# Four narrow bias tables moved from ScalarE to VectorE, and the wide tables placed earlier in ScalarE's order

## What is computed

```python
scores = scale * np.matmul(q, k.transpose(0, 1, 3, 2))       # B=2, H=8, S=768, D=64
keep = is_global | is_local                                  # first 8 keys, or 0 <= rel < 96
dist = np.where(is_global & ~is_local, float(n_local), np.abs(rel).astype(np.float32))
slopes = 2.0 ** (-8.0 * (np.arange(H) + 1) / H)
scores = scores - slopes[:, None, None] * dist               # then masked, softmax, times v
# x = attention output as (B, S, 512)
# block 1: u = x + (U V mixing over tokens); y = u + relu(u @ w_ch1) @ w_ch2
# block 2: h = relu(y @ w_in); half of it normalised, mixed over tokens, gated; @ w_out
```

## Time and profile before

| | |
|---|---|
| median of 3 runs | 502.89 us (502.85 to 502.91) |
| the profiled execution's own time | 502.92 us |
| its span, first to last instruction | 501.1 us |
| TensorE busy | 494.3 us, 99% of the span |
| VectorE busy | 284.9 us, 57% |
| ScalarE busy | 215.1 us, 43% |
| GpSimd busy | 209.3 us, 42% |
| granted TensorE clock, mean | 1.000 |

### The profile page before, as it was taken

How to read it: one execution, slowest core, us unless ns; L and a number is a source line. 1 busy time by engine, 2 the same in 40 slices (tenths; PEclk the granted TensorE clock), 3 DMA queues, 4 the chain that set the end, 5 groups by cost and what they waited for, 6 DMA issues and landing times.

```text
span 501.1 us, 7892 instructions
## 1 busy us (share of the span) xinstructions
PE 494.3 (99%) x2822; PEld 414.0 (83%) x2822; DVE 284.9 (57%) x666; ACT 215.1 (43%) x502; POOL 209.3 (42%) x178
## 2 busy tenths in 40 slices
PE   8999999999999999999999999999999999999997
PEld 7787677887888888888888888888888998889995
DVE  5887788521279466556574655648687356521530
ACT  7988789532334634232441331424655113321121
POOL 6797675443336765763666626513430000000000
PEclk9999999999999999999999999999999999999999
DMA  8721710132222322102222022021400000110002
GB/s 242 271 76 28 270 44 2 45 125 85 84 86 84 127 84 86 60 23 85 84 85 84 1 84 67 21 94 50 159 1 1 1 0 22 43 64 0 1 23 104
DMA packets 14553, 36.29 MB, mean 72 GB/s; under 512 B 2480, under 2 KB 2480, under 8 KB 14512
## 3 DMA queue, kind: packets, MB, share of 16 engines
q1 hardware_dynamic: 12640, 32.35, 19.4%
q10 hardware_dynamic: 1872, 3.41, 1.8%
HBM read 32.61 MB, written 3.15 MB: 71 GB/s over the span
## 4 chain that ended last, share of the span: by engine, by line
PE 94%; ACT 4%; DMA 1%; issue 1%; DVE 0%; SPq 0%; ACTq 0%
PE bank L1227 23%; PE bank L1498 15%; PE bank L1430 9%; PE bank L1358 9%; PE bank L1527 9%; PE bank L1520 9%; PE bank L1560 7%; PE bank L1283 4%; PE bank L1265 4%; PE bank L1250 3%; ACT prob L954 2%; PE bank L1297 1%; PE bank L1305 1%; DMA qk_raw<-in_qk 1%; PE bank L1330 1%; PE bank L1319 1%
## 5 line engine op out<-in xcount | busy, mean ns | idle before, releaser
L469 POOL TENSOR_TENSOR w_slot<-stage,w_slot 128x1024 fp32r<-128x1024 f32 x30 | 73.4, 2456 | 64.8 <-ACT w_slot L1024 64.8
L786 DVE TENSOR_TENSOR uT<-bank,uT 128x512 f32<-128x512 f32 x68 | 45.8, 689 | 25.2 <-PE bank L1527 23.2
L1227 PE MATMUL bank<-sp_slot,vn 128*128 128x384 f32 x288 | 50.3, 334 | 0.0
L1227 PEld LDWEIGHTS bank<-sp_slot,vn 128*128 128x128 f32 x288 | 50.0, 188 | 0.2
L954 ACT ACTIVATE prob<-prob,row_min 128x256 f32<-128x256 f32 (+1 forms) x96 | 45.9, 480 | 8.8 <-DVE row_min L604 8.7
L1498 PE MATMUL bank<-u_op,s_slot 128*128 128x512 f32 x192 | 47.6, 389 | 0.0
L1430 PE MATMUL bank<-hid,w_slot 128*128 128x512 f32 x192 | 46.9, 393 | 0.0
L1358 PE MATMUL bank<-u_split,w_slot 128*128 128x512 f32 x192 | 46.5, 391 | 0.0
L1527 PE MATMUL bank<-hid,w_slot 128*128 128x512 f32 x192 | 46.1, 389 | 0.0
L1520 PE MATMUL bank<-hid,w_slot 128*128 128x512 f32 x192 | 46.1, 389 | 0.0
L1430 PEld LDWEIGHTS bank<-hid,w_slot 128*128 128x128 f32 x192 | 35.7, 188 | 8.2 <-issue 0.9
(11 more groups left out here) (121 smaller groups left out, 837.5 us busy)
## 6 DMA issues: line engine op xcount, KB each, us to landing
stage<-in_w_ch SPq DMA_DIRECT2D x32, 512.0 KB, 3.3
qk_raw<-in_qk SPq DMA_DIRECT2D x23, 256.0 KB, 4.5
v_all<-in_v SPq DMA_DIRECT2D x12, 256.0 KB, 5.1
out_dram<-o_stage ACTq DMA_DIRECT2D x12, 256.0 KB, 2.0
stage<-in_w_spT SPq DMA_DIRECT2D x6, 384.0 KB, 3.0
stage<-in_w_in SPq DMA_DIRECT2D x4, 512.0 KB, 4.0
stage<-in_w_out SPq DMA_DIRECT2D x2, 512.0 KB, 3.5
V_raw<-in_V SPq DMA_DIRECT2D x4, 96.0 KB, 4.4
```

Of the source, the lines that this page charges most:

```text
L469: nc.gpsimd.tensor_tensor(dst[:, LO, :], stage[n % 2][:, 0:w], dst[:, HI, :].bitcast(F32), ALU.subtract).then_inc(w_lo, 1)
L786: vec.tensor_tensor(y, y_bank(e)[:], y, ALU.add).then_inc(y_sum, 1)
L1227: last = mm(out_ap, lhs(a), rhs(c), start=(n == 0), stop=(n == 3 * len(terms) - 1))
```

## The change

The change has three parts.

- VectorE makes the four narrow tables of heads 4 to 7, right behind the subtract at L587 and ahead of its register loads and branch, and counts a new semaphore, `bias0_far`. It waits for `dist0_set`, its own count.
- ScalarE makes only the narrow tables of heads 0 to 3. VectorE's `score_bias(0)` waits for `bias0_set`, `score_bias(1)` for `bias0_far`.
- ScalarE's wide pairs move: heads 0 to 3 ahead of `exps(0)`, heads 4 and 5 behind `exps(1)`, heads 6 and 7 ahead of `exps(2)`, and none ahead of `exps(3)`.

```diff
@@ vector, behind the subtract of the first tile @@
+            dve.wait_ge(dist0_set, 1)
+            for h in range(H // 2, H):
+                vec.tensor_scalar(bias0[:, h, :], dist0[:], -(2.0 ** -(h + 1)) / SCALE, None,
+                                  ALU.mult).then_inc(bias0_far, 1)
...
-                    if g < 2:
+                    if g == 0:
                         dve.wait_ge(bias0_set, heads(g, m)[1][1] + 1)
+                    elif g == 1:
+                        dve.wait_ge(bias0_far, heads(g, m)[1][1] + 1 - H // 2)
                     elif g < 4:
                         dve.wait_ge(bias_set, heads(g, m)[1][1] + 1)
@@ scalar @@
             act.wait_ge(dist0_set, 1)
-            for h in range(H):
+            for h in range(H // 2):
                 sc.activation(bias0[:, h, :], dist0[:], ACT.Copy, scale=-(2.0 ** -(h + 1)) / SCALE
                               ).then_inc(bias0_set, 1)
...
-                    if s in (-2, 0, 1):
-                        set_bias((0, None, 4, 6)[s + 2])
+                    if s == -2:
+                        set_bias(0)
+                        set_bias(2)
+                    if s == 0:
+                        set_bias(6)
...
                     if 0 <= s + 2 < QUADS:
                         exps(s + 2)
                     if s == -1:
-                        set_bias(2)
+                        set_bias(4)
```

More of the change, by code:

```diff
@@ L166, in build @@
         z_some, z_copy = sem("z_some"), sem("z_copy")
-        dist0_set, bias0_set = sem("dist0_set"), sem("bias0_set")
+        dist0_set, bias0_set, bias0_far = sem("dist0_set"), sem("bias0_set"), sem("bias0_far")
         bias_set, iotas, ident_set, V_split = sem("bias_set"), sem("iotas"), sem("ident_set"), sem("V_split")
```

## The result

| | before | after |
|---|---|---|
| median of 14 runs | 502.81 us (502.65 to 502.93) | 503.68 us (503.57 to 505.41) |
| ratio | | 1.002, 95% interval 1.0011 to 1.0028 |
| profiled execution, span | 502.92, 501.1 | 504.50, 502.7 |

The change makes the kernel 0.87 us slower. The interval of the ratio lies above 1, though the step is under the 1.0 us that the prediction took as the least that a measurement can tell. Forecast was 503.84 from the profiled execution before, 503.8 from its median.

The account below looks back on a forecast made before the run. A ScalarE-bound head of 18.44 us was taken to shift the TensorE-bound rest: 502.92 - 0.64 (wide tables' new places) + 1.56 (multiplies stopped by GpSimd) = 503.84, 503.8 from the median; range 502.1 to 504.4.

Parts of the forecast that it names:

- The head decides: First 18.44 us are bound by ScalarE; whatever moves the handover to TensorE at 18.44 moves the whole rest with it.
- ScalarE ready at 8.34, the branch takes 0.19: ScalarE before the first exponential: of 0.8 us taken away, 0.61 pays for the pair moved forward, 0.19 goes to the branch.
- The gain of 0.64: Behind quad 2 on ScalarE: no wide pair ahead of quad 3's exponentials, so weigh(2)'s second half starts at 17.80, not 18.44.
- The cost of 1.56: VectorE's four multiplies take turns with GpSimd, so the first score row (L604) starts at 9.31 instead of 7.75.
- Who is first at 7.6: GpSimd's subtract wants its turn at 7.61, VectorE's third multiply at 7.67: GpSimd goes first, by 0.06 us.
- The second rival: Three multiplies get in ahead of GpSimd's subtract, L604 starts at 8.75: cost 1.00, time 503.25; chance 0.15.
- the third: GpSimd gets its turn after every multiply, L604 at 10.68: cost 2.93, time 505.2; chance 0.12 with its milder form (503.95).
- The bounds: Multiplies against a busy GpSimd: between running free, as L868 did, and being fully stopped, as L870 was.
- The first rival: Multiplies don't stop for GpSimd and L604 moves by 0 to 0.1: time 502.3; chance 0.22.
- what I don't see: Chance 0.08 left for the tables' earlier place gaining nothing (504.4) and for TensorE's longer idle time ahead of turn(0).

Follow-up runs that it names:

- the subtract held back: Changed kernel, with GpSimd's first subtract (L430) waiting until VectorE's four multiplies are counted: 502.30, and 502.18 when run again.
- the order alone: Changed kernel with only the new places of the wide tables; ScalarE makes all eight narrow tables, VectorE none: 502.82, ratio 0.9995.
- more fill: Changed kernel with fill(11) instead of fill(5) ahead of the first transposes: 503.69, and 503.73 when run again.
- two multiplies: Changed kernel with two narrow tables (heads 6 and 7) on VectorE and six on ScalarE: 502.34 when run again, ratio 0.9979.
- the tables alone: Changed kernel with the four narrow tables on VectorE but the wide pairs in their old places: 504.41, ratio 1.0026.
- the PSUM source: Changed kernel, with VectorE's four multiplies reading a PSUM copy of the distance table, one copy added: 503.19, a median between two groups.
- three multiplies: Changed kernel with three narrow tables (heads 5 to 7) on VectorE and five on ScalarE: 503.15, ratio 1.0009.
- the register loads first: Kernel before, with VectorE's two register loads of the configuration moved ahead of its two L587: 506.07, ratio 1.0053.

## Why the prediction was right

**The head decides.** Right. The chain passes from ScalarE to TensorE at 19.29 instead of 18.44, 0.85 later, and the execution is 0.8 longer in span (501.9 against 501.1), so nearly all of it is left at the end.

**ScalarE ready at 8.34, the branch takes 0.19.** Right: the four wide tables start at 6.99, 0.09 after the last narrow one ends, and end at 8.33.

**The gain of 0.64.** Right in size and place. The distance from the first exponential to the copy of probT(2) was forecast at 8.87 and measured at 8.84 in the changed kernel, 8.84 with the subtract held back, 8.82 with the order alone. The wait on bias_set ahead of quad 3's second scores, which the profile had called "issue", is gone from VectorE's rows.

**The cost of 1.56.** Right: the score row moved by 9.29 - 7.75 = 1.54. The ends of the four multiplies were forecast at 7.46, 7.60, 8.83 and 9.39 and came at 7.45, 7.59, 8.82 and 9.37. The step that I was least sure of, that these multiplies with one input stop for GpSimd, is shown by three runs: it goes when GpSimd's subtract is held back (502.2), it goes in steps with the number of multiplies, and it goes when the source is PSUM. The Trainium skill's rule ("SBUF — State Buffer", section "SBUF: two separate sides") names the two-port mode beside two-input instructions; this case's trace agrees for both, as far as a multiply that took 0.13 us for 128 columns is in that mode, with 1.31 us for one that took 0.21 when it was free. That the reading rate is the reason was argued in the prediction and isn't shown apart from the source: out of PSUM the multiplies also are slower, 0.20 apart instead of 0.13, and no run has one that reads SBUF at the lower rate.

**Who is first at 7.6.** Forecast by a margin of 0.06 us, and it held in every profile of four multiplies out of SBUF in which both L587 went ahead of the cast and the subtract wasn't held back (four of them, multiplies together 2.54 or 2.55); in the one laid out above the subtract started at 7.46 and took its turn ahead of the third multiply. A margin that small is a narrow call, and the prediction gave it 0.43 and no more. It also took one step for granted: that both L587 always go ahead of GpSimd's cast. In two profiles, with more fill and with two multiplies, they don't (last section). The second rival (three get through, 503.25) and the third (one in every gap, 505.2) hung on that margin. The third was not empty: the profiled execution at 504.99 has an order near it (below), by the step just named and not by the margin at 7.6.

**The bounds.** The first rival, 502.3, was the right time for the kernel in which the cause is taken away: 502.18 and 502.30.

**The distribution.** Where I was short: executions above 504.4, the upper end of the range, are five of 22 of the changed kernel, three of fourteen and two of eight. I had left 0.08 for what I don't see and named TensorE's idle time in it. Two of the five (504.50, 505.93) show a lower mean granted clock, 0.997 and 0.996; the other three (504.79, 505.41, 505.42) weren't profiled.

## What to carry to other kernels

Idle time of an engine isn't free room when its work would share something with a neighbour that is busy in it: before moving small elementwise work into VectorE's gap, lay GpSimd's rows of the same microsecond beside it and write down the order of ends. If the moved work reads two columns a cycle or two SBUF tensors, either keep the number that fits between two GpSimd instructions, or hold back the GpSimd instruction, if it has slack (0.54 us of it bought 1.5 us here). And an edit that has a cost and a gain is worth being taken apart: the order alone gave 0, the tables alone +1.5, both with one wait -0.7. Where a time falls in two groups, read the granted clock of each execution before the mean or the median is explained.

## What the runs showed of the hardware that I had not expected

**The order of turns isn't the same in every execution.** The kernel with more fill, profiled at 504.99, had the granted clock at 1.00 in all of its head, and was late for another reason:

```profile
5.81 1.70 DVE L587 TENSOR_TENSOR qk_split<-qk_raw,qk_split 128x512 fp32r<-128x512 f32 x2
7.44 3.20 DVE L593 TENSOR_SCALAR bias<-dist 128x128 f32<-128x128 f32 x4
...
6.34 0.63 POOL L428 CAST qk_split<-qk_raw 128x512 fp32r<-128x512 f32 x1 [3.88 <-DMA qk_raw<-in_qk]
7.05 1.60 POOL L430 TENSOR_TENSOR qk_split<-qk_raw,qk_split 128x512 fp32r<-128x512 f32 x1
```

Here VectorE's L587 started 0.53 ahead of GpSimd's cast, and the cast (0.63, unhindered) got in between the two L587; in the execution at 503.69 it started 0.64 ahead, and both L587 went first. With the tables alone 0.59 ahead was enough as well. Both starts hang on the landing of DMAs, of the configuration for L587 and of q and k for the cast. From there everything is turned by one place: the multiplies take 3.20 and end at 10.64. So a shift of 0.1 us in a landing moves this kernel by over 1 us (504.99 against 503.69). The profiled execution with two multiplies at 505.47 has the same order (L587 at 5.83, the cast at 6.27, both L587 in 1.70), but it was late for the reason that comes next.

**TensorE's rows in the executions at 505.3 to 505.8.** Three of them were profiled: with the subtract held back (505.45), with the tables alone (505.49) and with two multiplies (505.47). In all three the chain runs over TensorE from 6.2 or 6.6 us to 14.7 or 14.8. In the first two the order of turns is the usual one, so the turns aren't the cause. Here are the same stretch and the same instructions in the kernel before and then with the subtract held back:

```profile
6.20:14.70 8.50, 8.30 (x91) 6.80 (x92) 6.74 (x37) 8.47 (x39) 8.15 (x10) 1.00 1.07 328
...
6.37 1.58 PE L1250 MATMUL bank<-qk_split 64*128 64x128 f32 x24 [0.18 <-DVE qk_split L587]
7.88 1.38 PE L1219 MATMUL bank<-ident 128*128 128x128 f32 x10
```

```profile
6.20:14.70 8.50, 8.47 (x56) 7.86 (x58) 4.33 (x24) 6.70 (x30) 7.62 (x8) 1.00 1.07 333
...
6.23 2.82 PE L1263 MATMUL bank<-qk_split 64*128 64x128 f32 x24
8.98 2.50 PE L1232 MATMUL bank<-ident 128*128 128x128 f32 x10
```

The products take 1.8 times as long, 0.25 us each in the last line, about what the first twenty take in the same profiles (4.64 from 1.54 us on). The granted clock stands at 1.00 in both, so it doesn't tell these executions apart, and why they are slow is open. With TensorE as the bound it no longer matters what VectorE and ScalarE do there: kernels with medians from 502.2 to 504.4 all come out at 505.3 to 505.5. The kernel before has 13 such executions in 107 (505.45 to 505.76). None of them was profiled; that they are of this kind is likely by their time, not shown.

**TensorE's clock in the head.** In the changed kernel's first profile the order of turns was the usual one (multiplies ending at 7.38, 7.51, 8.74 and 9.29), and it was late by the clock. First that execution (504.50), then the one at 503.69, the same stretch:

```profile
11.80:15.60 3.80, 3.80 (x28) 2.90 (x27) 2.64 (x12) 3.80 (x18) 2.74 (x4) 0.56 1.05 345
```

```profile
11.80:15.60 3.80, 3.76 (x44) 2.82 (x44) 3.20 (x14) 3.80 (x18) 2.93 (x5) 1.00 1.03 355
```

TensorE was idle for 1.57 us ahead of its first transposes in the one and for 1.23 us in the other, and only in the first did its clock go down to the lower level (1.2 GHz), where the same twelve products of scores(2) took 1.33 instead of 0.98:

```profile
11.81 1.33 PE L1261 MATMUL bank<-qk_split 64*128 64x256 f32 x12
```

```profile
11.89 0.98 PE L1261 MATMUL bank<-qk_split 64*128 64x256 f32 x12
```

That is worth 0.8 us (504.50 against 503.69). Other executions with a mean granted clock of 0.997, those with the register loads first aside, lie at 503.6 to 504.1: five of twelve with the PSUM source, two of twelve with three multiplies, one each with two multiplies and with the order alone, two of the kernel before. Whether the idle time causes it is open. The clock also fell in the profile with the PSUM source, where TensorE had been idle for 0.63 and 0.33 us just before, less than the 1.23 us after which it stayed up. Of 23 executions with more fill none has a mean under 0.999, and of 22 of the changed kernel two have; that is too few to tell. The four late ones with more fill are at 1.00, and the profiled one of them was late by the order of turns.

**What stands behind register loads waits.** ScalarE's and VectorE's loads of the configuration run ahead of work that is already queued, as the earlier trace rows show, but work behind them isn't started until they are done: L588 at 6.25, with loads at 5.3 and 5.9 us (0.55 and 0.32).
